# Block-masked Jacobi, identities added in VectorE's evictions, a one-product inverse, and another order of loads at the head

## The chip, the cores and the metric

One NeuronCore of a Trainium2 chip. Its engines are TensorE (PE; PEld is its weight load), VectorE (DVE), ScalarE (ACT), GpSimd (POOL) and SyncE (SP), each with its own queue of instructions in order, synchronised by semaphores. Time is device microseconds of one execution; lower is better.

## The reference

Three layers, one after the other, on 3072 tokens of width 384. The first is attention with a delta rule, 4 batches of 8 heads, 768 tokens, head dimension 48:

```python
k_n = k / (norm(k) + 1e-6)
for t in range(S):
    y[t] = q[t] @ state
    state = state + beta[t] * outer(k_n[t], v[t] - k_n[t] @ state)
```

Then a mixture of 8 experts (`argmax` of `x @ w_gate` picks one per token; `relu(x @ w1[e]) @ w2[e]`, scaled by a gate), and then `max(x @ w1, x @ w2, x @ w3) @ w_out` on every token.

## The kernel before

**Stages.** `attention_and_router` computes the delta rule, the router's logits and each token's place in a sorted list; `experts` runs over that list in tiles of 128 rows with a run-time number of tiles for each expert; `last_layer` runs over blocks of 512 rows.

**Attention in chunks.** The sequence is cut into chunks of 64 tokens. A step `k` (12 of them, `STEPS`) holds one pair of chunks for each of two streams (`st` 0 and 1, two batches), all 8 heads and two chunks at once: U = 8 blocks of 64x64 on each half of the partitions. For a chunk the recurrence is a triangular system, so each step and stream needs the inverse of I + a strictly triangular N of 64x64, for every head and chunk. It is made by the list `INV`:

- `kt`: transposes of the normalised keys; `gram`: products of keys with keys and queries (32 matmuls of 48x64 by 48x128), evicted by VectorE (L531) through `beta_mask` into `n_kb_a`; `split`: ScalarE casts N to 16 bits, `n_hi` (L483); `low`: GpSimd makes the rest, `n_lo` (L694).
- `jacobi` 0, 1, 2: T := mask(I + N T) within 4x4 blocks. TensorE (`diagonal`, L337) first puts the identity into PSUM with one pair of 64x512 matmuls, then sixteen 64x64 matmuls (`each_head`, L330) add N T; VectorE evicts through a mask (L535).
- `turn`: T transposed (ScalarE evicts, L486), and T put into the accumulator. `prod` and `update` 2 to 5: four doublings of the block size; VectorE evicts `p16` through a level's mask (L538), ScalarE evicts T and its transpose (L489, L491).
- `resid`: 2 pairs of `diagonal` (I and -T) and 32 small matmuls give I - T + N T, evicted by ScalarE (L494) to `p16`; `inv`: sixteen matmuls that copy T, transposed, into PSUM, a wait, and sixteen that add the correction; evicted by ScalarE to `t_inv` (L497).

`CHAIN` is what depends on the state of the chunk before: `ks`, `z`, `up` for each of two chunks, then `yt` (transpose), `lg` (logits, L454; VectorE copies them and picks the expert, L560 to L569), `rank` (L462, L463, the place among tokens of that expert), `slot`, and `send`, in which GpSimd scatters the rows of a tile to DRAM (L709).

**Order.** `walk` writes the order out by hand, the same for all engines: 16 slots per step; stream 1 runs `H` = 9 slots behind stream 0; `CHAIN` runs 17 slots behind `INV`. In slot 2 of step `k` stands stream 0's `split`, in slot 11 stream 1's. `NORM` prepares the keys of the next step: GpSimd squares them (`ksq`, L718), VectorE sums (L585), ScalarE takes roots (L517), VectorE inverts, GpSimd scales (`kn`, L685). Parts 10 to 12 convert a sixth of expert 0's weights each in steps 2 to 7 (L627, L638). Part 13, once, has GpSimd load expert 1's weights (L722).

**Queues at the head.** SyncE issues, in this order: keys of step 0 (`load_raw`, L274), `k_own` of step 0 (L279), `cf`, `beta`, `ch` (L289 to L291), queries and values of step 0, all loads of step 1, `wr` (L299), the first weights (L303), and the keys of step 2. TensorE, VectorE and GpSimd each wait for `const_in` 64, which the four constants make up together. In steps 2 to 11 SyncE also writes 14 blocks of zeros to `ys`, 192 KB each.

Of the kernel before, what the change touches and what calls it, by code (L numbers as in the profile page):

```python
# [16 lines left out]
P = 128  # L17
BATCH, HEADS, SEQ, D = 4, 8, 768, 48
DP = 64
C = 64  # L20
# [20 lines left out]
CF_IOTA = CF_BASE + C  # L41
# [8 lines left out]
CH_TRI = CH_REP + U * C  # L50
# [5 lines left out]
BLANK = MAXB - TILES  # L56
# [3 lines left out]
def constants():  # L60
# [10 lines left out]
    cf[:, CF_BASE:CF_BASE + C] = (row >> 2 == col >> 2) & (row >= col)  # L71
# [6 lines left out]
    ch[:, CH_REP:CH_REP + U * C] = np.tile(row == col, (1, U))  # L78
# [26 lines left out]
def attention_and_router(nc, ctx, sems, kt_in, kh, qh, vh, bh, cf_in, ch_in, wr_in, cf, ch, wr, routing, xs, ys, weights, w1, w2):  # L105
# [25 lines left out]
    n_lo = single("n_lo", [P, U, C], F16)  # L131
    t16 = single("t16", [P, U, C], F16)
# [10 lines left out]
    y_t = single("y_t", [P, KX, P], F32)  # L143
    best = sb("best", [P, 2], F32)
# [15 lines left out]
    const_in = sem("const_in")  # L160
    k_in = pair_of("k_in")
# [14 lines left out]
    n_lo_ready = pair_of("n_lo_ready")  # L176
    kb_ready = pair_of("kb_ready")
# [5 lines left out]
    updt_done = pair_of("updt_done")  # L183
    updtt_done = pair_of("updtt_done")
# [33 lines left out]
    ident_rep = ch[:, CH_REP:CH_REP + U * C]  # L218
# [8 lines left out]
    def mask_of(lv):  # L227

        at = CF_BASE if lv is None else CF_LV + (lv - LV0) * C
        return cf[:, at:at + C].unsqueeze(1).broadcast_to((P, U, C))  # L230
# [12 lines left out]
    NORM = {1: [0], 2: [1], 3: [2], 4: [10], 5: [3], 6: [4], 7: [5], 8: [6], 9: [7, 8], 10: [9], 12: [11], 13: [13], 14: [12]}  # L243
# [25 lines left out]
    def _(sp):  # L269
# [17 lines left out]
        for st in range(2):  # L287
            load_own(0, 0, st)
# [3 lines left out]
        for st in range(2):  # L292
            load_qv(0, 0, st)
        load_raw(1, 1)
# [22 lines left out]
        sp.wait_ge(zeroed, 16 * BLANK)  # L317
# [4 lines left out]
        sp.wait_ge(zeroed, 16 * BLANK + 16)  # L322

    @block.tensor
    def _(pe):
# [17 lines left out]
        def eye(s, u):  # L343
            return ident_rep[s, 0:C]

        def inv(k, par, st, what, lv):
            tb, ttb, pb = bank[st]
            n, nl, t, tt, pr = (lambda s, u, x=x[st]: x[s, u, :] for x in (n_hi, n_lo, t16, tt16, p16))
# [19 lines left out]
            elif what == "jacobi":  # L368
                if lv == 0:
                    pe.wait_ge(gram_out[st], 2 * k + 2)  # L370
                    pe.wait_ge(n_hi_ready[st], k + 1)
# [3 lines left out]
                diagonal(ident16, ident_rep, pb, True)  # L375
                each_head(n, eye if lv == 0 else t, pb).then_inc(jacobi_done[st], 1)
# [5 lines left out]
            elif what == "prod":  # L382
                if lv > LV0:
                    pe.wait_ge(t_out[st], LVS * k + lv - LV0)
                    pe.sem_inc(passed_pe, 1)
                each_head(n, t, pb, first=True).then_inc(prod_done[st], 1)
            elif what == "update":
# [3 lines left out]
                each_head(tt, pr, tb).then_inc(updt_done[st], 1)  # L391
                each_head(pr, tt, ttb).then_inc(updtt_done[st], 1)
            elif what == "resid":
# [3 lines left out]
                diagonal(ident16, ident_rep, pb, True)  # L397
                diagonal(neg16, flat(t16[st]), pb, False)
                each_head(n, t, pb)
                each_head(nl, t, pb).then_inc(resid_done[st], 1)  # L400
            elif what == "inv":
                pe.wait_ge(tt_out[st], (LVS + 1) * (k + 1))
                pe.sem_inc(passed_pe, 1)
                each_head(t, eye, ttb, first=True)
                pe.wait_ge(resid_out[st], k + 1)
                pe.sem_inc(passed_pe, 1)
                each_head(pr, tt, ttb).then_inc(inv_done[st], 1)

        def chain(k, par, st, what, e):
# [40 lines left out]
            elif what == "lg":  # L450
                pe.wait_ge(yt_out[st], k + 1)
                pe.sem_inc(passed_pe, 1)
# [13 lines left out]
        pe.wait_ge(const_in, 64)  # L466
# [7 lines left out]
    def _(act):  # L474
        def inv(k, par, st, what, lv):
# [11 lines left out]
            elif what == "update":  # L487
                act.wait_ge(updt_done[st], LVS * k + lv - LV0 + 1)
                act.copy(t16[st][:], tb).then_inc(t_out[st], 1)  # L489
                act.wait_ge(updtt_done[st], LVS * k + lv - LV0 + 1)  # L490
# [27 lines left out]

        act.wait_ge(blank, 1)
# [3 lines left out]
    def _(dve):  # L523
        def inv(k, par, st, what, lv):
# [8 lines left out]
            elif what == "jacobi":  # L533
                dve.wait_ge(jacobi_done[st], 3 * k + lv + 1)
                dve.tensor_tensor(t16[st][:], pb, mask_of(None), ALU.mult).then_inc(jacobi_out[st], 1)  # L535
            elif what == "prod":
                dve.wait_ge(prod_done[st], LVS * k + lv - LV0 + 1)
                dve.tensor_tensor(p16[st][:], pb, mask_of(lv), ALU.mult).then_inc(prod_out[st], 1)  # L538
# [41 lines left out]
        def norm(k, par, part):  # L580
# [26 lines left out]
            elif part == 9:  # L607
                dve.wait_ge(inv_norm, k + 1)
                if k >= 2:
# [42 lines left out]
        dve.wait_ge(const_in, 64)  # L652
        dve.tensor_copy(counted[:], ch[:, CH_AREA:CH_AREA + E])
# [24 lines left out]
    def _(pool):  # L678
        def inv(k, par, st, what, lv):
# [7 lines left out]
            elif what == "mask":  # L687
                if k >= 1:
                    pool.wait_ge(gram_out[st], 2 * k)
                pool.tensor_tensor(beta_mask[st][:], gp_mask.unsqueeze(1).broadcast_to((P, U, 2, C)),  # L690
                                   b.unsqueeze(2).unsqueeze(3).broadcast_to((P, U, 2, C)), ALU.mult).then_inc(beta_ready[st], 1)
            elif what == "low":
# [10 lines left out]
        def chain(k, par, st, what, e):  # L703
            if what == "send":
                to = 2 * k + st
                pool.wait_ge(slot_ready[st], k + 1)
                if k >= 1:
                    pool.wait_ge(rows_sent[st], 16 * k)
                pool.indirect_dma_start(xs, bass.IndirectOffsetOnAxis(ap=rows_at[:, to:to + 1], axis=0),  # L709
                                        y_tile[par][st][:], None).then_inc(rows_sent[st], 16)  # L710

        def norm(k, par, part):
# [6 lines left out]
            elif part == 13 and k == STEPS - 2:  # L719
                for i, w in enumerate((w1, w2)):  # L720
                    pool.wait_ge(weights.lo_ready[i], 1)
# [605 lines left out]
```

## Time and profile before

| | us |
|---|---|
| median of 3 runs | 1129.34 |
| lowest, highest | 1124.27, 1130.99 |
| the profiled execution | 1126.3 |
| its span, first to last instruction | 1124.6 |

| engine | busy us | share |
|---|---|---|
| TensorE matmul | 1025.3 | 91% |
| VectorE | 522.9 | 46% |
| ScalarE | 366.1 | 33% |
| GpSimd | 311.2 | 28% |

Attention runs from the head to about 510 us, the experts to about 860, the last layer to the end. Busy time on TensorE includes the drain of a matmul, which the next one overlaps; the distance between two starts is the better measure. A wait in brackets behind a row is idle time of that engine before it, with what ended it.

### The profile page before, as it was taken

The numbers are of one execution on the slowest core, as the hardware profiler recorded it, in microseconds if no ns is written. First come the engines' busy times: TensorE is split into PE (matmuls) and PEld (weight loads), VectorE is DVE, ScalarE is ACT, GpSimd is POOL, SyncE is SP. The second block draws the span as 40 slices with busy tenths as digits, with TensorE's granted clock in tenths as the row PEclk, the third lists the DMA queues.
The fourth block names the chain that finished last, engine by engine and source line by source line (L and its number), as shares of the span: only waits on it lengthen the run. The fifth ranks groups of instructions, "written<-read, shape, count | busy, mean of one in ns | idle before, by whom it ended". The sixth has DMA issues, their size and how long they took to land. (4 is left out here: it accounts for less than half of the span.)

```text
span 1124.6 us, 30958 instructions
## 1 busy us (share of the span) xinstructions
PE 1025.3 (91%) x13260; PEld 894.7 (80%) x13260; DVE 522.9 (46%) x1134; ACT 366.1 (33%) x730; POOL 311.2 (28%) x202
## 2 busy tenths in 40 slices
PE   0789989989999899975999999999599999999998
PEld 0677878878888788864999999998488888888888
DVE  4456666766666565525443444434242423232221
ACT  0245455545555455531222222222121212212111
POOL 2423433333334232103254555226310100000000
PEclk9999999999999999976999999999699999999999
DMA  8012122212221512002444344233201010100000
GB/s 273 16 31 77 41 73 66 70 56 84 62 79 40 196 34 64 17 15 93 154 167 169 130 160 152 105 124 115 72 27 36 22 43 14 42 21 22 15 15 29
DMA packets 58263, 84.90 MB, mean 75 GB/s; under 512 B 29088, under 2 KB 53024, under 8 KB 55584
## 3 DMA queue, kind: packets, MB, share of 16 engines
q1 hardware_dynamic: 52480, 46.94, 13.4%
q0 software_dynamic: 5664, 36.18, 9.4%
q8 instruction: 98, 1.61, 0.6%
q14 instruction: 21, 0.17, 0.1%
HBM read 61.67 MB, written 21.43 MB: 74 GB/s over the span
## 5 line engine op out<-in xcount | busy, mean ns | idle before, releaser
L1077 PE MATMUL hb<-early,last_h 128*128 128x512 f32 x648 | 208.2, 403 | 1.2 <-DVE early L1209 1.2
L1077 PEld LDWEIGHTS hb<-early,last_h 128*128 128x128 f32 x648 | 121.8, 191 | 29.4 <-DVE early L1209 1.6
L1077 PE MATMUL hb<-early,last_l 128*128 128x512 f32 x324 | 129.3, 399 | 0.0
L1215 DVE TENSOR_TENSOR m<-hb,m 128x512 f32<-128x512 f32 x36 | 24.9, 692 | 132.5 <-PE hb L1077 132.5
L330 PEld LDWEIGHTS bank<-t,n_hi 64*64 64x64 f16 x2688 | 65.9, 111 | 24.0 <-issue 8.5
L538 DVE TENSOR_TENSOR p<-bank,cf 128x512 f16<-128x512 f32 x96 | 66.0, 688 | 30.5 <-PE bank L330 29.6
L330 PE MATMUL bank<-t,n_hi 64*64 64x64 f16 x2688 | 72.7, 196 | 4.6 <-issue 3.7
L1077 PE MATMUL ob<-wo_h,early 128*128 128x384 f32 x288 | 75.2, 339 | 0.0
L1077 PEld LDWEIGHTS hb<-early,last_l 128*128 128x128 f32 x324 | 61.7, 190 | 15.1
L999 POOL TENSOR_TENSOR late<-w_raw,late 128x3072 fp32r<-128x3072 f32 x8 | 54.5, 6811 | 57.8 <-DVE late L939 57.5
L535 DVE TENSOR_TENSOR t<-bank,cf 128x512 f16<-128x512 f32 x72 | 49.7, 691 | 40.7 <-PE bank L330 40.0
L908 ACT CAST ht_h<-ht_bank 128x512 fp32r<-128x512 f32 x56 | 32.9, 587 | 109.3 <-PE ht_bank L862 55.4
L1110 POOL DMA_INDIRECT rows<-y_sorted,idx x24 | 23.0, 959 | 159.3 <-DVE scaled L1205 156.1
L489 ACT CAST t<-bank 128x512 f16<-128x512 f32 x96 | 56.3, 586 | 28.3 <-PE bank L330 26.2
L926 DVE TENSOR_TENSOR ht_l<-ht_bank,ht_h 128x512 fp32r<-128x512 f32 x56 | 38.7, 691 | 56.7 <-ACT ht_h L908 56.2
L790 PE MATMUL y_acc<-early,ht_h 128*128 128x384 f32 x240 | 63.8, 347 | 0.0
L709 POOL DMA_INDIRECT x_sorted<-y_tile,rows_at x24 | 24.4, 1017 | 128.7 <-DVE rows_at L577 127.3
L790 PE MATMUL h_bank<-early,xt_h 128*128 128x512 f32 x180 | 58.5, 407 | 1.4 <-DVE xt_l L921 1.3
L440 PE MATMUL chain<-z,n_kb_a 128*128 128x96 f32 x384 | 55.3, 287 | 3.4 <-issue 3.4
L491 ACT CAST tt<-bank 128x512 f16<-128x512 f32 x96 | 56.9, 593 | 0.9 <-PE bank L330 0.9
L685 POOL TENSOR_TENSOR kn<-k_raw,nrm 128x384 f32<-128x384 f32 x24 | 20.0, 834 | 133.2 <-DVE nrm L606 132.9
L421 PE MATMUL chain<-state,kq_t 128*128 128x96 f32 x384 | 55.2, 288 | 1.8 <-issue 1.6
(162 smaller groups left out, 2203.8 us busy)
## 6 DMA issues: line engine op xcount, KB each, us to landing
w_raw<-w POOLq DMA_DIRECT2D x14, 1536.0 KB, 7.6
kq_t<-qh SPq DMA_DIRECT2D x24, 256.0 KB, 3.4
y_sorted<-y_sb SPq DMA_DIRECT2D x31, 192.0 KB, 1.9
x_in<-x_sorted SPq DMA_DIRECT2D x29, 192.0 KB, 2.7
k_raw<-kt_in SPq DMA_DIRECT2D x24, 192.0 KB, 3.4
k_own<-kh SPq DMA_DIRECT2D x24, 192.0 KB, 3.2
v_in<-vh SPq DMA_DIRECT2D x24, 192.0 KB, 3.8
out<-o_sb SPq DMA_DIRECT2D x24, 192.0 KB, 1.8
```

What stands on the lines that cost most here:

```text
L330: ins = pe.matmul(out[s, C * u:C * u + C], lhs(s, u), rhs(s, u), start=first and u == 0, stop=True, skip_group_check=True)
L421: ins = pe.matmul(out[:, W * p:W * p + W], kq_t[par][st][:, NP * e + p, :, :].rearrange("q a t -> q (a t)"), state[st][:, p].rearrange("q ...
L440: ins = pe.matmul(out[:, W * p:W * p + W], n_kb_a[par][st][:, NP * e + p, 1:3, :].rearrange("q a t -> q (a t)"), z[st][:, p].rearrange("q ...
L489: act.copy(t16[st][:], tb).then_inc(t_out[st], 1)
L491: act.copy(tt16[st][:], ttb).then_inc(tt_out[st], 1)
L535: dve.tensor_tensor(t16[st][:], pb, mask_of(None), ALU.mult).then_inc(jacobi_out[st], 1)
L538: dve.tensor_tensor(p16[st][:], pb, mask_of(lv), ALU.mult).then_inc(prod_out[st], 1)
L790: ins = pe.matmul(out, a[x], b[y], start=first and i == 0, stop=last and i == 2)
L908: act.copy(ht[0][:, 4 * n:4 * n + 4].rearrange("p c t -> p (c t)"), ht_bank[n][:, :]).then_inc(ht_hi[n], 1)
L926: dve.tensor_tensor(ht[1][:, 4 * n:4 * n + 4].rearrange("p c t -> p (c t)"), ht_bank[n][:, :], ht[0][:, 4 * n:4 * n + 4].rearrange("p c t ...
L999: pool.tensor_tensor(splits[par][i][1], weights.flat_raw(i), splits[par][i][0], ALU.subtract).then_inc(weights.lo_ready[i], 1)
L1077: ins = pe.matmul(out, a[x], b[y], start=first and i == 0, stop=last and i == 2, skip_group_check=True)
```

## The change

- **Head.** `load_own` of step 0 goes behind the queries and values. `wr` gets a semaphore of its own, which only the first `lg` waits for, and `const_in` is waited for up to 48. GpSimd waits at its start for neither constants nor `blank`; its first `mask` waits for the constants. VectorE's wait for the constants and its copy into `counted` move to part 9 of step 0. ScalarE takes the root of a zero before anything else, so that its table is loaded.
- **Zeros.** The 14 writes to `ys` become one, issued ahead of the first weights. `BLANK` goes.
- **Expert 1's weights** are loaded by GpSimd behind the send of tile 22 (last step, stream 0) and no longer in part 13 of step 10.
- **Jacobi.** In `split`, GpSimd multiplies N by the mask of 4x4 blocks into a new 16-bit tile, `n_base`; the three rounds use it, without the identity products; VectorE's eviction adds the identity (from `cf`) and does not mask. `n_hi` is first waited for by `prod` 2. `CF_BASE` is the whole block mask.
- **Residual and inverse.** `resid` leaves out the identity product; VectorE, not ScalarE, evicts it and adds 2 I. `inv` is one set of sixteen products, of (2 I - T + N T) and T, without those that copied T.

```diff
@@ constants
+CF_EYE, CF_TWO: I and 2 I, 64 columns each; CH_REP shrinks from U*C to C columns
-    cf[:, CF_BASE:CF_BASE + C] = (row >> 2 == col >> 2) & (row >= col)
+    cf[:, CF_BASE:CF_BASE + C] = row >> 2 == col >> 2
...
@@ SyncE
         load_raw(0, 0)
-        for st in range(2):
-            load_own(0, 0, st)
         sp.dma_start(cf[:], cf_in).then_inc(const_in, 16)
         sp.dma_start(beta[:], bh).then_inc(const_in, 16)
         sp.dma_start(ch[:], ch_in).then_inc(const_in, 16)
         for st in range(2):
             load_qv(0, 0, st)
+        for st in range(2):
+            load_own(0, 0, st)
...
-        sp.dma_start(wr[:], wr_in).then_inc(const_in, 16)
+        sp.dma_start(wr[:], wr_in).then_inc(wr_in_sbuf, 16)
         sp.wait_ge(zeros_ready, 1)
+        sp.dma_start(ys[P * (LEAD + TILES):P * (LEAD + MAXB), :].rearrange("(n p) x -> p n x", p=P),
+                     zeros[:].unsqueeze(1).broadcast_to((P, MAXB - TILES, X))).then_inc(zeroed, 16)
...
-            for i in range(BLANK * (k - 2) // (STEPS - 2), BLANK * (k - 1) // (STEPS - 2)):
-                at = P * (LEAD + TILES + i)
-                sp.dma_start(ys[at:at + P, :], zeros[:]).then_inc(zeroed, 16)
@@ TensorE
             elif what == "jacobi":
                 if lv == 0:
                     pe.wait_ge(gram_out[st], 2 * k + 2)
-                    pe.wait_ge(n_hi_ready[st], k + 1)
+                    pe.wait_ge(n_base_ready[st], k + 1)
...
-                diagonal(ident16, ident_rep, pb, True)
-                each_head(n, eye if lv == 0 else t, pb).then_inc(jacobi_done[st], 1)
+                each_head(nb, eye if lv == 0 else t, pb, first=True).then_inc(jacobi_done[st], 1)
...
             elif what == "resid":
...
-                diagonal(ident16, ident_rep, pb, True)
-                diagonal(neg16, flat(t16[st]), pb, False)
+                diagonal(neg16, flat(t16[st]), pb, True)
                 each_head(n, t, pb)
                 each_head(nl, t, pb).then_inc(resid_done[st], 1)
             elif what == "inv":
                 pe.wait_ge(tt_out[st], (LVS + 1) * (k + 1))
-                pe.sem_inc(passed_pe, 1)
-                each_head(t, eye, ttb, first=True)
                 pe.wait_ge(resid_out[st], k + 1)
                 pe.sem_inc(passed_pe, 1)
-                each_head(pr, tt, ttb).then_inc(inv_done[st], 1)
+                each_head(pr, tt, ttb, first=True).then_inc(inv_done[st], 1)
...
-        pe.wait_ge(const_in, 64)
+        pe.wait_ge(const_in, 48)
@@ ScalarE
-            elif what == "resid":
-                act.wait_ge(resid_done[st], k + 1)
-                act.copy(p16[st][:], pb).then_inc(resid_out[st], 1)
...
+        act.wait_ge(zeros_ready, 1)
+        act.activation(root_of_zero[:], zeros[:, 0:1], ACT.Sqrt)
@@ VectorE
-                dve.tensor_tensor(t16[st][:], pb, mask_of(None), ALU.mult).then_inc(jacobi_out[st], 1)
+                dve.tensor_tensor(t16[st][:], pb, of_heads(CF_EYE), ALU.add).then_inc(jacobi_out[st], 1)
+            elif what == "resid":
+                dve.wait_ge(resid_done[st], k + 1)
+                dve.tensor_tensor(p16[st][:], pb, of_heads(CF_TWO), ALU.add).then_inc(resid_out[st], 1)
...
             elif part == 9:
                 dve.wait_ge(inv_norm, k + 1)
+                if k == 0:
+                    dve.wait_ge(const_in, 48)
+                    dve.tensor_copy(counted[:], ch[:, CH_AREA:CH_AREA + E])
@@ GpSimd
+            elif what == "split":
+                pool.wait_ge(gram_out[st], 2 * k + 2)
+                pool.tensor_tensor(n_base[st][:], n_kb_a[par][st][:, :, 0, :], of_heads(CF_BASE), ALU.mult).then_inc(n_base_ready[st], 1)
...
                                         y_tile[par][st][:], None).then_inc(rows_sent[st], 16)
+                if to == TILES - 2:
+                    for i, w in enumerate((w1, w2)):
+                        pool.wait_ge(weights.lo_ready[i], 1)
+                        pool.dma_start(weights.raw[i][:], w[1]).then_inc(weights.raw_again[i], 16)
...
-            elif part == 13 and k == STEPS - 2:
...
-        pool.wait_ge(const_in, 64)
-        pool.wait_ge(blank, 1)
```

## Rows read from the trace of the kernel before

**Rows 1.** A window of attention: length, busy of PE, PEld, DVE, ACT, POOL, PEclk, DMA.

```profile
235.00:265.00 30.00, 28.98 (x725) 25.10 (x720) 21.68 (x51) 16.08 (x35) 9.45 (x8) 1.00 0.28 80
```

**Rows 2.** Timeline of all engines, 0 to 50 us: start, us, engine, line, operation.

```profile
0.89 0.88 SPq L274 DMA_DIRECT2D k_raw<-kt_in  x2
...
14.99 0.43 SPq L299 DMA_DIRECT2D wr<-wr_in  x1
...
18.57 1.47 POOL L718 TENSOR_TENSOR ksq<-k_raw 128x768 f32<-128x768 f32 x1 [17.99 <-DMA wr<-wr_in]
...
21.11 1.28 ACT L517 ACT_TABLE_LOAD   x1 [21.11 <-DVE nrm L585]
...
25.19 1.08 PE L353 MATMUL bank<-cf,kn 128*128 128x128 f32 x4 [25.19 <-POOL kn L685]
...
27.05 3.67 PE L365 MATMUL bank<-kq_t 48*64 48x128 f32 x32 [0.77 <-ACT kq_t L479]
```

**Rows 3.** DMA of 0 to 25 us: traffic, then issues with KB and us to landing.

```profile
DMA packets 6739, 7.44 MB, mean 298 GB/s; under 512 B 4566, under 2 KB 6230, under 8 KB 6486
...
k_raw<-kt_in SPq DMA_DIRECT2D x5, 192.0 KB, 2.5
...
ch<-ch_in SPq DMA_DIRECT2D x1, 258.0 KB, 5.9
```

**Rows 4.** Timeline of VectorE: the key sums of three steps.

```profile
289.32 0.94 DVE L585 TENSOR_REDUCE nrm<-ksq 128x16 f32<-128x768 f32 x1
...
361.27 0.94 DVE L585 TENSOR_REDUCE nrm<-ksq 128x16 f32<-128x768 f32 x1
...
403.19 0.94 DVE L585 TENSOR_REDUCE nrm<-ksq 128x16 f32<-128x768 f32 x1
```

**Rows 5.** Timeline of TensorE in one step, 200 to 235 us.

```profile
205.66 0.38 PE L337 MATMUL bank<-ch 64*64 64x512 f16 x2
205.88 0.41 PE L330 MATMUL bank<-t,n_hi 64*64 64x64 f16 x16
206.22 0.84 PE L454 MATMUL chain<-wr,y_t 128*128 128x16 f32 x6
206.99 0.44 PE L330 MATMUL bank<-ch,t 64*64 64x64 f16 x16
207.27 0.42 PE L330 MATMUL bank<-tt,p 64*64 64x64 f16 x16
...
208.78 0.17 PE L462 MATMUL chain<-chosen,ch 128*128 128x8 f16 x1 [0.37 <-DVE chosen L569]
```

**Rows 6.** Timeline of all engines around stream 1's first Jacobi round.

```profile
195.99 1.96 PE L365 MATMUL bank<-kq_t 48*64 48x128 f32 x32
...
197.19 1.50 DVE L531 TENSOR_TENSOR n_kb_a<-bank,beta_mask 128x512 f32<-128x512 f32 x2 [0.40 <-PE bank L365]
...
200.63 0.63 ACT L483 CAST n_hi<-n_kb_a 128x512 f16<-128x512 f32 x1
...
201.35 1.15 POOL L694 TENSOR_TENSOR n_lo<-n_kb_a,n_hi 128x512 f16<-128x512 f32 x1 [4.49 <-ACT n_hi L483]
201.36 0.40 PE L337 MATMUL bank<-ch 64*64 64x512 f16 x2 [0.43 <-issue]
```

**Rows 7.** Windows around the load of expert 1's weights (columns as in Rows 1).

```profile
385.00:390.00 5.00, 1.73 (x45) 1.51 (x38) 0.69 (x1) 1.17 (x3) 1.90 (x2) 1.00 0.99 402
390.00:395.00 5.00, 4.83 (x102) 4.17 (x101) 2.18 (x8) 1.06 (x2) 0.00 (x0) 0.62 0.44 122
```

**Rows 8.** Timeline of all engines, 379 to 393 us.

```profile
390.18 0.35 PE L440 MATMUL chain<-z,n_kb_a 128*128 128x96 f32 x2 [3.44 <-issue]
```

**Rows 9.** Timeline of GpSimd: the send of tile 22.

```profile
498.23 0.97 POOL L709 DMA_INDIRECT x_sorted<-y_tile,rows_at  x1 [9.58 <-DVE rows_at L577]
```

**Rows 10.** Instructions on `w_raw`, 60 to 540 us: ns min/median/max, first and last start.

```profile
L939 DVE CAST late<-w_raw x2: 1760/2382/3003, 521.2 to 528.6; 128x3072 fp32r<-128x3072 f32 x2
...
DMA to landing us min/median/max: 7.0/7.8/11.2
```

More of the change, by code:

```diff
@@ L40 @@
 CF_BASE = CF_LV + (LEVELS - 2) * C
-CF_IOTA = CF_BASE + C
+CF_EYE = CF_BASE + C
+CF_TWO = CF_EYE + C
+CF_IOTA = CF_TWO + C
 CF_STEP = CF_IOTA + E
@@ L49 @@
 CH_REP = CH_NEG + P
-CH_TRI = CH_REP + U * C
+CH_TRI = CH_REP + C
 CH_ONE = CH_TRI + P
@@ L55 @@
 LEAD = 3
-BLANK = MAXB - TILES
 AREA = TILES + MINB
@@ L70, in constants @@
         cf[:, CF_LV + (lv - 2) * C:CF_LV + (lv - 1) * C] = below & ((col >> lv) == (row >> lv) - 1)
-    cf[:, CF_BASE:CF_BASE + C] = (row >> 2 == col >> 2) & (row >= col)
+    cf[:, CF_BASE:CF_BASE + C] = row >> 2 == col >> 2
+    cf[:, CF_EYE:CF_EYE + C] = row == col
+    cf[:, CF_TWO:CF_TWO + C] = 2.0 * (row == col)
     cf[:, CF_IOTA:CF_IOTA + E] = E - np.arange(E)
@@ L77, in constants @@
     ch[:, CH_NEG:CH_NEG + P] = -np.eye(P)
-    ch[:, CH_REP:CH_REP + U * C] = np.tile(row == col, (1, U))
+    ch[:, CH_REP:CH_REP + C] = row == col
     ch[:, CH_TRI:CH_TRI + P] = np.arange(P)[:, None] < np.arange(P)[None]
@@ L131, in attention_and_router @@
     n_lo = single("n_lo", [P, U, C], F16)
+    n_base = single("n_base", [P, U, C], F16)
     t16 = single("t16", [P, U, C], F16)
@@ L160, in attention_and_router @@
     const_in = sem("const_in")
+    wr_in_sbuf = sem("wr_in_sbuf")
     k_in = pair_of("k_in")
@@ L176, in attention_and_router @@
     n_lo_ready = pair_of("n_lo_ready")
+    n_base_ready = pair_of("n_base_ready")
     kb_ready = pair_of("kb_ready")
@@ L225, in attention_and_router, with of_heads @@
     rows = [slice(C * hh, C * hh + D) for hh in range(2)]
-    def mask_of(lv):
-        at = CF_BASE if lv is None else CF_LV + (lv - LV0) * C
+    def of_heads(at):
         return cf[:, at:at + C].unsqueeze(1).broadcast_to((P, U, C))
@@ L343, in eye @@
         def eye(s, u):
-            return ident_rep[s, 0:C]
+            return eye16[s, :]
         def inv(k, par, st, what, lv):
             tb, ttb, pb = bank[st]
-            n, nl, t, tt, pr = (lambda s, u, x=x[st]: x[s, u, :] for x in (n_hi, n_lo, t16, tt16, p16))
+            n, nl, nb, t, tt, pr = (lambda s, u, x=x[st]: x[s, u, :] for x in (n_hi, n_lo, n_base, t16, tt16, p16))
             if what == "kt":
@@ L384, in inv @@
                     pe.wait_ge(t_out[st], LVS * k + lv - LV0)
-                    pe.sem_inc(passed_pe, 1)
+                else:
+                    pe.wait_ge(n_hi_ready[st], k + 1)
+                pe.sem_inc(passed_pe, 1)
                 each_head(n, t, pb, first=True).then_inc(prod_done[st], 1)
@@ L451, in chain @@
                 pe.wait_ge(yt_out[st], k + 1)
+                if k == 0 and st == 0:
+                    pe.wait_ge(wr_in_sbuf, 16)
                 pe.sem_inc(passed_pe, 1)
@@ L718, in norm @@
                 pool.tensor_tensor(ksq[:], keys, keys, ALU.mult).then_inc(squares, 1)
-            elif part == 13 and k == STEPS - 2:
-                for i, w in enumerate((w1, w2)):
-                    pool.wait_ge(weights.lo_ready[i], 1)
-                    pool.dma_start(weights.raw[i][:], w[1]).then_inc(weights.raw_again[i], 16)
-        pool.wait_ge(const_in, 64)
-        pool.wait_ge(blank, 1)
         run(lambda a, c, b, n: walk(a, c, b, n, inv, chain, norm))
```

29 lines of the change are left out of this document (14 added, 15 removed).

## The prediction

> **What bounds the kernel now.** I read the page's engine shares first, then the windows of 30 us through the attention stage, then the timeline of all engines at the head, the timeline of TensorE inside one steady step, and the waits that are left. The page gives TensorE 91% of the span (table above), and a window in the middle of attention has it busy for 28.98 of 30 us, VectorE 21.68, ScalarE 16.08 [rows 1]. So TensorE sets the pace there, and what an edit is worth is the distance between starts on TensorE, not the printed duration: a group of sixteen 64x64 matmuls prints 0.41 to 0.44 us but the next one starts 0.28 to 0.34 us later [rows 5]. At the head it is otherwise: nothing is multiplied until 25.19 us, because GpSimd's first square waits 17.99 us for the last of the constant loads, `wr`, issued at 14.99 behind the data of steps 0 and 1 [rows 2]. From there the work is one dependent chain. The third thing is a single hole: at 390.18 TensorE had waited 3.44 us inside a group of matmuls for nothing that the profile names ("issue"), while the DMA engines were 0.99 busy, and afterwards the clock stood at a mean of 0.62 for 5 us [rows 7, 8], a mix of its levels 1.2 and 2.4 GHz.
>
> **The head.** Two loads of keys are issued by 1.77 us [rows 2] and land a median 2.5 us later [rows 3], so about 4.3; the added freedom is that GpSimd waits for nothing else. Before, the first square began at 18.57 and the first transpose at 25.19, 6.62 us of chain. The table load of the root, 1.28 us of it, now runs while the keys arrive (zeros are written early, ScalarE is idle). That leaves 5.34 us: TensorE could start at 4.3 + 5.3 = 9.6. It also waits for three constants now: their issues (0.43 us each, as the row of `wr` has it) follow the keys at once, so the last, `ch`, is issued near 3.2 and lands 5.9 us later [rows 3], at about 9.1, in time. I take 9.9 us, a gain of 15.3; bounds 12 (constants late behind traffic, 13 us) to 16.
>
> **What that start runs into.** Up to 25 us the queue moved 7.44 MB at a mean of 298 GB/s [rows 3]. One write of 14 x 192 KB = 2.75 MB of zeros is added ahead of the first weights (and taken from later steps): 9.2 us more at that rate, so the DMA engines are full until about 34 us, and the first inversion now runs under that, from 10 us. Its data (queries, values, the keys of step 1) are issued ahead of the zeros, the keys of step 2 are wanted a whole step later. What can suffer is TensorE's own instruction supply. The nearest row is the hole of 3.44 us under a full DMA [rows 8]; the chain is sparse here, since it waits for evictions, so I charge 2 us, bounds 0 and 7 (two such holes).
> The Trainium skill (Runtime: NRT & Kernel Launch, Instruction fetch mechanics) says that instructions come in blocks by the sequencer's own DMA queue and that crossing a block is mostly hidden. By that rule this term would be 0; the row of 3.44 us speaks for a cost when the engines are full.
>
> **The weights of expert 1.** Their two loads leave the tenth step and go behind the send of tile 22, at 498.23 before [rows 9]; they land 7.0 to 11.2 us after issue, so by about 510, and VectorE first reads them at 521.2 [rows 10]. What follows them on GpSimd's queue is only the last send. Cost 0 to 2 us if that send lands late, I take 0.5. What goes is the hole: the marks of VectorE's key sums stand at 289.32, 361.27 and 403.19 [rows 4]: two steps of 35.98 and then one of 41.92, so the step with the loads cost 5.9 more. I take all of it; bounds 3 and 6. The remaining zero writes also leave the steps, one or two of 192 KB each; I take 2 us for shorter refill holes, bounds 0 and 6.
>
> **The inversion on TensorE.** Per step and stream: each of three Jacobi rounds loses a pair of 64x512 products with the identity, the residual loses one such pair, and the inverse loses the sixteen products that copied T. A pair takes 205.88 - 205.66 = 0.22 us of TensorE's order, the sixteen 207.27 - 206.99 = 0.28 us [rows 5]. That is 4 x 0.22 + 0.28 = 1.16 us, and with 12 steps and 2 streams 27.8 us. Not all of it is the end's to have:
> - The sixteen stand between the logit products and the rank product, which at 208.78 waits for VectorE's choice of expert (0.37 us [rows 5]). VectorE's work from the logits on is not shorter, so what is taken ahead of the wait only lengthens it. I count these 0.28 at nothing: 24 x 0.28 = 6.7 us lost, 21.1 left.
> - The residual's eviction moves from ScalarE to VectorE; two evictions take 1.50 there [rows 6], so 0.75 us more, twice a step, on an engine busy 21.68 of 30 [rows 1]. What is queued behind it is the third Jacobi eviction and then the logits' copy, whose choice the rank product waits for. In the steps with weight pieces I charge 0.5, in the others 0.1: 3.5 us in all; bounds 0 and 0.75 x 24 = 18.
> - The Jacobi rounds take a masked N that GpSimd makes (1.15 us, by the row of n_lo, an operation of the same size) where ScalarE's copy took 0.63 [rows 6]. But ScalarE got to it late: in stream 1 the masked Gram was ready at 197.19 + 1.50 = 198.69, the copy ran at 200.63, and TensorE stood 0.43 us [rows 6]. GpSimd can start at once (its next task is queued behind): 198.8 + 1.15 = 199.95, ahead of TensorE's arrival near 200.9. That takes away about 0.6 us of distance in eleven steps, 6.6 us. In stream 0 the two paths come out equal. A GpSimd that is late by a mask or a send would lose 1 to 2 us a step instead; bounds: gain 7, loss 12; I take a gain of 4.
> - Additions in the evictions cost what the multiplications by a mask did: same engine, same operands.
>
> So attention gains 21.1 - 3.5 + 4 = 21.6 us in the stage; in the first chain, where latency counts, the pairs leave too and GpSimd's 0.5 us longer mask comes in, which is within these numbers. Behind attention nothing is changed but the counts of a semaphore.
>
> **The sum** is 15.3 - 2 + 5.9 - 0.5 + 2 + 21.6 = 42.3 us. The profiled execution took 1126.3 us (its span is 1124.6); less the sum, 1084.0. The median of the runs is 1129.34, 3 us above; the same sum from there is 1087.0. I put the forecast between, at 1086. About 1% (11 us) is what a measurement of this kernel can tell from no change.
>
> **Rivals.**
> - *TensorE's time goes, but the waits take it.* With VectorE busy 21.68 of 30 us and every eviction in order behind another, the stage could keep its steps: only 8 us of the 21.6 come through. Then 1126.3 - 15.3 + 2 - 5.9 - 8 - 1.5 = 1098. For it: only a few waits in a steady step are at zero margin, and they are VectorE's; against it: groups follow each other at their shortest distance nearly everywhere.
> - *The full DMA at the head starves the first chain.* Two or three holes of 3.44 us and late constants: the head yields 5 instead of 13.3, giving 1094; for it the row of the hole, against it that before, too, loads were behind loads and landed in 2.5 to 5.9 us.
> - *The holes and the clock's dips were worse than counted.* If the refill holes leave with the zeros and no dip follows, and TensorE's 27.8 us come through whole: about 1071.
> - *Slower: the clock.* The head already shows the lower level: 32 Gram products took 3.67 us at 27.05 [rows 2] against 1.96 at 195.99 [rows 6], half rate, while TensorE waited for evictions; and after the hole it fell again [rows 7]. The change removes the widest products and leaves the waits. If TensorE fell to 1.2 GHz in attention, a step of 36 us with 29/30 of it on TensorE would grow by up to 35 us; 1.2 such steps, one in ten, eat the whole sum, and three give 1126.3 - 42.3 + 105 = 1189. Against it: a window of 28.98 busy us of 30 held the level 1.00 [rows 1], and 2 us less of a 36 us step leave it at nine tenths.
> The Trainium skill (TensorE: Matmul & The Clock Gate, HAM oscillation) warns of just this: idle stretches between products send the engine to half rate. The trace agrees after the hole; whether shorter waits suffice, no row of the steady steps shows.
>
> **Chances.** The forecast's case (1076 to 1093) 0.56, waits take it (1093 to 1106) 0.16, a starved head 0.12, better than counted (1066 to 1076) 0.11, the clock or something that turns it around 0.05, of which 0.02 land within 1%. Range 1069 to 1104: it takes in a starved head and most of the waits, and leaves out the tails of both sides. Faster by over 1% (under 1118) 0.95, within 1% 0.02, slower 0.03.
>
> **What would show it.** The first transpose near 10 us and no later than 13; the key-sum marks of VectorE 34 to 35 us apart with no step near 42; no 64x512 identity pair in the Jacobi rounds; the first Jacobi group without a wait on stream 1; the rank product waiting longer (0.6 us or more) than 0.37; the first read of expert 1's weights without a wait. A mark spacing still over 36 us would say that the waits took the gain; Gram groups of 3.7 us outside the first 40 us would say the clock.

## The result, and the profile after

The changed kernel takes 1169.64 us (median of 4, 1159.48 to 1184.01) against 1130.16 us: a ratio of 1.032, interval 1.021 to 1.044. It is slower; the forecast was 1086, and the whole range 1069 to 1104 lay on the wrong side. One of the four, 1184.01 us, was a slow execution, and the mean of the other three is 1166.3, so differences from this kernel are known to about 13 us only. The profiled execution has a span of 1157.3 us.

The page of the changed kernel: span, busy time of two engines in 40 slices, the granted clock in tenths, and the group of GpSimd's new operation.

```profile
span 1157.3 us, 29818 instructions
...
PE   4798878988989989984999999999599999999999
...
DVE  5666776776766767643544344344242314242321
...
PEclk9977888887799989986899999999789999999999
...
L703 POOL TENSOR_TENSOR n_base<-n_kb_a,cf 128x512 f16<-128x512 f32 x24 | 30.8, 1284 | 199.4 <-DVE n_kb_a L534 199.4
```

The clock is what leaps out: under nine tenths in most slices of attention (the first 19), where TensorE has 576 matmuls fewer. The head did what it should. Timeline of all engines, the lines that answer to [rows 2]:

```profile
3.90 1.47 POOL L734 TENSOR_TENSOR ksq<-k_raw 128x768 f32<-128x768 f32 x1 [3.31 <-DMA k_raw<-kt_in]
...
9.31 1.09 PE L357 MATMUL bank<-cf,kn 128*128 128x128 f32 x4 [9.31 <-POOL kn L692]
```

15.9 us earlier than before. All of that is given back, and more, between 50 and 440 us: the third key sum comes at 49.18 us (62.79 before), the twelfth at 435.55 (403.19 before), so that 46 us are lost between them. Some of VectorE's key sums, which answer to [rows 4]:

```profile
227.06 0.94 DVE L591 TENSOR_REDUCE nrm<-ksq 128x16 f32<-128x768 f32 x1
...
271.64 0.94 DVE L591 TENSOR_REDUCE nrm<-ksq 128x16 f32<-128x768 f32 x1
...
319.05 0.94 DVE L591 TENSOR_REDUCE nrm<-ksq 128x16 f32<-128x768 f32 x1
...
359.34 0.94 DVE L591 TENSOR_REDUCE nrm<-ksq 128x16 f32<-128x768 f32 x1
...
394.99 0.94 DVE L591 TENSOR_REDUCE nrm<-ksq 128x16 f32<-128x768 f32 x1
```

Steps of 44.6, 47.4, 40.3 and 35.7 us, where the same four took 38.1, 36.2, 36.5 and 35.4 before. Windows of 50 us (busy of PE, PEld, DVE, ACT, POOL, then the clock; columns as in [rows 1]):

```profile
100.00:150.00 50.00, 43.34 (x877) 38.31 (x877) 34.30 (x74) 19.35 (x41) 15.51 (x13) 0.77 0.17 48
...
250.00:300.00 50.00, 43.80 (x861) 38.89 (x856) 34.82 (x74) 18.99 (x41) 16.62 (x14) 0.76 0.16 44
...
350.00:400.00 50.00, 46.21 (x1097) 41.19 (x1098) 35.94 (x88) 24.97 (x55) 19.91 (x18) 0.97 0.18 53
```

A mean of 0.76 is half the time at 1.2 GHz and half at 2.4. The one step of 35.7 us lies where the clock held (1.00 from 359 to 395 us). So two questions: what made TensorE wait, and what the clock adds.

The timeline of all engines (weight loads left out), right behind stream 1's Gram products, answers to [rows 6]:

```profile
203.87 1.94 PE L369 MATMUL bank<-kq_t 48*64 48x128 f32 x32
...
205.07 1.49 DVE L534 TENSOR_TENSOR n_kb_a<-bank,beta_mask 128x512 f32<-128x512 f32 x2
...
206.47 3.34 DVE L626 TENSOR_TENSOR beta_k<-nrm,beta 64x8 f32<-64x8 f32 x4
206.63 1.30 POOL L703 TENSOR_TENSOR n_base<-n_kb_a,cf 128x512 f16<-128x512 f32 x1 [3.77 <-DVE n_kb_a L534]
...
207.89 1.90 POOL L699 TENSOR_TENSOR beta_mask<-cf,beta 128x1024 f32<-128x1024 f32 x1
...
208.62 0.42 PE L334 MATMUL bank<-ch,n_base 64*64 64x64 f16 x16
...
209.84 0.71 DVE L561 TENSOR_TENSOR state<-state,chain 64x192 f32<-64x192 f32 x2
...
210.65 0.52 PE L450 MATMUL chain<-cf,y_tile 128*128 128x128 f32 x3 [1.61 <-issue]
...
211.42 0.44 PE L334 MATMUL bank<-p,tt 64*64 64x64 f16 x16 [0.25 <-DVE p L544]
```

GpSimd makes the masked N at once, as forecast, and the first Jacobi group starts without a wait. But VectorE's next work is `beta_k`, four products of 64x8 elements from two SBUF tiles, 0.17 us each when alone. Here the four take 3.34 us: they end when GpSimd's mask of N and then `beta_mask`, which stands behind it, have ended (207.89 + 1.90 = 209.79). In the kernel before the same four took 0.68 us, because GpSimd had made that `beta_mask` well ahead of the Gram's eviction:

```profile
193.80 1.90 POOL L690 TENSOR_TENSOR beta_mask<-cf,beta 128x1024 f32<-128x1024 f32 x1
...
198.60 0.68 DVE L617 TENSOR_TENSOR beta_k<-nrm,beta 64x8 f32<-64x8 f32 x4
```

The new operation waits for VectorE's eviction of the Gram (3.77 us in the row at 206.63), and all that GpSimd has behind it in its queue now runs beside what VectorE does next. In the changed kernel the state's update waits behind `beta_k`, `yt` waits for the state, and TensorE stands 1.61 us (put down to "issue", but VectorE's row at 209.84 is what it needed) and 0.25 more. The groups of VectorE that were held, over attention, changed kernel:

```profile
L626 DVE TENSOR_TENSOR beta_k<-nrm,beta 64x8 f32<-64x8 f32 x48 | 39.3, 818 | 0.5
...
L636 DVE CAST early<-w_raw 128x512 fp32r<-128x512 f32 x12 | 19.7, 1682 | 0.0
L647 DVE TENSOR_TENSOR early<-w_raw,early 128x512 fp32r<-128x512 f32 x12 | 17.1, 1423 | 0.0
```

and the kernel before:

```profile
L638 DVE TENSOR_TENSOR early<-w_raw,early 128x512 fp32r<-128x512 f32 x12 | 15.0, 1247 | 0.0
...
L617 DVE TENSOR_TENSOR beta_k<-nrm,beta 64x8 f32<-64x8 f32 x48 | 11.1, 232 | 0.5
...
L627 DVE CAST early<-w_raw 128x512 fp32r<-128x512 f32 x12 | 4.5, 418 | 0.0
```

VectorE loses 28.2 + 15.2 + 2.1 = 45.5 us by being held. The Trainium skill (SBUF — State Buffer, Who interferes with whom) states the rule: an instruction of VectorE with two SBUF inputs contends with one of GpSimd that reads SBUF, and a copy or cast in a two-port mode contends with GpSimd too; whichever is issued first has the shared ports for the whole instruction, and the other is blocked. The trace agrees: 0.68 us for four against 3.34, and 0.42 us for a cast against 1.68.

### The profile page after: what moved, and what is told of

Read it like the earlier page. It is cut to its first block and busy times, and to the rows that moved or that the text cites. A ratio compares the mean times of both kernels' runs of the same rounds, so it can differ in the third digit from the quotient of the medians.

```text
span 1157.3 us, 29818 instructions
## 1 busy us (share of the span) xinstructions
PE 1043.1 (90%) x12684; PEld 917.5 (79%) x12684; DVE 579.5 (50%) x1158; ACT 353.6 (31%) x707; POOL 340.3 (29%) x226
## 5 line engine op out<-in xcount | busy, mean ns | idle before, releaser
L703 POOL TENSOR_TENSOR n_base<-n_kb_a,cf 128x512 f16<-128x512 f32 x24 | 30.8, 1284 | 199.4 <-DVE n_kb_a L534 199.4
L423 PE MATMUL chain<-state,kq_t 128*128 128x96 f32 x384 | 67.3, 330 | 0.9 <-issue 0.4
L553 DVE TENSOR_TENSOR rhs<-v_in,chain 64x192 f32<-64x192 f32 x96 | 33.4, 348 | 68.4 <-PE chain L423 66.9
L334 PEld LDWEIGHTS bank<-t,n_hi 64*64 64x64 f16 x1920 | 51.2, 119 | 19.0 <-issue 12.8
L918 ACT CAST ht_h<-ht_bank 128x512 fp32r<-128x512 f32 x56 | 32.9, 587 | 109.3 <-PE ht_bank L872 55.4
L334 PE MATMUL bank<-tt,p 64*64 64x64 f16 x1920 | 57.9, 203 | 7.4 <-issue 7.2
L334 PE MATMUL bank<-t,n_hi 64*64 64x64 f16 x1920 | 58.4, 205 | 5.3 <-issue 3.6
L423 PEld LDWEIGHTS chain<-state,kq_t 128*128 128x128 f32 x384 | 59.6, 237 | 2.8 <-issue 1.2
L442 PE MATMUL chain<-z,n_kb_a 128*128 128x96 f32 x384 | 60.5, 306 | 0.0
L538 DVE TENSOR_TENSOR t<-bank,cf 128x512 f16<-128x512 f32 x72 | 49.4, 686 | 22.0 <-PE bank L334 21.4
```

Of the source, the lines that this page charges most:

```text
L334: ins = pe.matmul(out[s, C * u:C * u + C], lhs(s, u), rhs(s, u), start=first and u == 0, stop=True, skip_group_check=True)
L423: ins = pe.matmul(out[:, W * p:W * p + W], kq_t[par][st][:, NP * e + p, :, :].rearrange("q a t -> q (a t)"), state[st][:, p].rearrange("q ...
L442: ins = pe.matmul(out[:, W * p:W * p + W], n_kb_a[par][st][:, NP * e + p, 1:3, :].rearrange("q a t -> q (a t)"), z[st][:, p].rearrange("q ...
L538: dve.tensor_tensor(t16[st][:], pb, of_heads(CF_EYE), ALU.add).then_inc(jacobi_out[st], 1)
L553: dve.tensor_tensor(rhs[st][s, :, hh, :], v_in[par][st][s, e], by_head[0:C, hh], ALU.subtract).then_inc(rhs_out[st], 1)
L918: act.copy(ht[0][:, 4 * n:4 * n + 4].rearrange("p c t -> p (c t)"), ht_bank[n][:, :]).then_inc(ht_hi[n], 1)
```

## The experiments

Theory P: GpSimd's added operation holds VectorE up, and TensorE waits. Theory C: without the identity products TensorE does too little and its clock falls. All medians below were taken beside runs of the kernel before, at 1127.6 to 1129.2 us.

**Head and moves alone**

```diff
  the head, the zeros and the load of expert 1's weights as in the change; the inversion as before
```

> The kernel before with the new head, the one write of zeros and the later load of expert 1's weights; the inversion as before. Both theories (P: GpSimd's new mask of N holds VectorE up through two-input operations; C: TensorE loses its clock because the identity products are gone) say that nothing of the loss is here: first transpose near 9.3 us (15.9 less), the step with the 3.44 us hole 6 less, clock as before: 1130 - 20 = 1106 to 1112 us. A third theory, H (the early, sparse start and the full DMA bring the clock down), says above 1130.

1107.66 us, ratio 0.979 (0.973 to 0.985). So nothing of the loss is here, H is out, and the terms of the sum for these parts, 20.7 us, hold together: 21.5. Not each of them does; see the section on the prediction. This kernel is the base of the next ones.

**Jacobi alone**

```diff
  base, and
-                diagonal(ident16, ident_rep, pb, True)
-                each_head(n, eye if lv == 0 else t, pb).then_inc(jacobi_done[st], 1)
+                each_head(nb, eye if lv == 0 else t, pb, first=True).then_inc(jacobi_done[st], 1)
  GpSimd's n_base, VectorE's eviction + I
```

> The head and moves as in the run beside it, and of the inversion only the Jacobi part: GpSimd's masked N, no identity products in the three rounds, identity added in VectorE's eviction; residual and inverse as before. P: VectorE's beta_k operations take 0.7 us each as in the changed kernel and the time is near that of it, 1150 to 1170. C: three of the four pairs are gone, so most of the clock loss too, 1150 to 1170, but with beta_k back at 0.25 us. If it is the residual's eviction on VectorE (theory V): 1090 to 1100.

1173.79 us, 66 above the base and no faster than the whole change. `beta_k` took 0.80 us each, so this is P, with or without C. The loss is all in the Jacobi part.

**Residual and inverse alone**

```diff
  base, and the residual evicted by VectorE with 2 I, one pair and the sixteen copy products out
```

> The kernel of 1107.66 us, with only the residual and the inverse changed: one pair and the sixteen copy products less, the residual evicted by VectorE. P: GpSimd has nothing new, so 1098 to 1107. C: one pair less of four: 1100 to 1115. If the eviction on VectorE is what costs (V): 1115 to 1125.

1104.02 us, 3.6 below the base, with both at some us of spread: no loss, and little of the 24 x (0.22 + 0.28) = 12 us that TensorE was spared. V is out. (The prediction's terms for this part are 24 x 0.22 - 3.5 = 1.8 us.)

**GpSimd's operation alone**

```diff
  base, and
+            elif what == "split":
+                pool.wait_ge(gram_out[st], 2 * k + 2)
+                pool.tensor_tensor(n_base[st][:], n_kb_a[par][st][:, :, 0, :], base mask, ALU.mult)
```

> The kernel of 1107.66 us, with only GpSimd's masked copy of N added, which nothing reads and nobody waits for; TensorE's work as before. P: VectorE's beta_k goes from 0.19 to 0.8 us, TensorE waits 1 to 4 us more in each step and the time is 1135 to 1165. C, or that it is the Jacobi rounds' wait for GpSimd: no change, 1105 to 1112.

1147.33 us: 39.7 us for an operation that nobody waits for, 24 times. Groups of VectorE:

```profile
L626 DVE TENSOR_TENSOR beta_k<-nrm,beta 64x8 f32<-64x8 f32 x48 | 38.5, 802 | 0.5
L636 DVE CAST early<-w_raw 128x512 fp32r<-128x512 f32 x12 | 19.6, 1676 | 0.0
```

P is shown without any edit on TensorE. But the clock fell here too, with all the identity pairs in place. A window of 50 us:

```profile
100.00:150.00 50.00, 45.10 (x954) 39.11 (x956) 34.37 (x74) 21.01 (x44) 15.50 (x13) 0.81 0.18 49
```

In the four windows from 50 to 250 us it was 0.93, 0.81, 0.85 and 0.83, which is 58 us at 1.2 GHz. So up to 29 of the 39.7 us can be the clock's, brought down by the waits. Under "Jacobi alone" the mask is made by GpSimd as well, but three of the four pairs are out and the rounds wait for the mask: there 16 us less of work on TensorE went with 26 us more of time.

**The same, with `beta_k` moved**

```diff
-    NORM = {... 9: [7, 8], 10: [9], 12: [11], 13: [13], 14: [12]}
+    NORM = {... 9: [7, 8], 12: [11], 14: [12], 15: [9]}
```

> The 1147.33 us kernel (old inversion, GpSimd makes a masked N that nobody reads), with beta_k moved from slot 10 to 15. If the collision with beta_k is what it costs: beta_k at 0.2 us and 1108 to 1120 (1107.66 without the extra operation; the weight casts are still held in steps 2 to 7). If the extra operation costs by its presence: above 1130.

1126.44 us (median of ten; one of them took 2457.6 us, the others 1122.11 to 1130.78), 21 of the 40 us back, less than expected. The clock of the profiled run went from 0.946 to 0.971. The rest lies in the steps with weight pieces:

```profile
L647 DVE TENSOR_TENSOR early<-w_raw,early 128x512 fp32r<-128x512 f32 x12 | 22.9, 1905 | 0.0
L636 DVE CAST early<-w_raw 128x512 fp32r<-128x512 f32 x12 | 19.6, 1675 | 0.0
L626 DVE TENSOR_TENSOR beta_k<-nrm,beta 64x8 f32<-64x8 f32 x48 | 9.2, 192 | 0.5
```

The casts stay held and the remainders even more (1.91 us for 1.19 in the base). By VectorE's key sums five of these six steps take 41 to 42 us and the later ones 35.4 to 36.3. So the collisions, with `beta_k` and with the weight pieces, are the cost. That the operation's presence alone is not, the run called "Both" below shows best: there GpSimd makes the mask, all collisions are moved and the pairs stand, and the time is 1108.52 us, 0.9 above the base (it is spared the sixteen copy products, which with a pair were worth 3.6 us in the run above).

**The change, with `beta_k` moved**

```diff
  the changed kernel with part 9 of NORM in slot 15
```

> The changed kernel (1169.64 us), with only beta_k moved from slot 10 to slot 15; the weight casts stay at 4, 12 and 14. P, and mostly by beta_k (39.3 us of the 45 that VectorE lost): beta_k back at 0.2 us, 1130 to 1145, most of the 40 us that all the shifts gave. If the casts count as much: 1145 to 1160, and in the steps without weight pieces no change against the run with all shifts.

1126.57 us: one small group, moved by five slots, gives 43 us (40 from the mean of 1166.3). It is more than expected. The clock of the profiled run is 0.950, against 0.926.

**The change, with all colliding operations moved**

```diff
-    NORM = {... 4: [10], ... 8: [6], 9: [7, 8], 10: [9], 12: [11], 14: [12]}
+    NORM = {... 8: [6, 10], 9: [7, 8], 14: [11], 15: [12, 9]}
```

> The changed kernel, with VectorE's operations that read two SBUF tiles or copy from SBUF moved to slots in which GpSimd has run out of work: beta_k from slot 10 to 15, the weight casts from 4 to 8, the weight remainders from 12 and 14 to 14 and 15. Nothing is added to TensorE. P: beta_k falls from 0.8 to 0.2 us, the clock comes back to 0.97 and the time to 1085 to 1105. C: VectorE is freed but the clock still falls in ten places: 1140 to 1165.

1129.75 us, neither theory's number, and no better than with `beta_k` alone, though the casts are back at 0.42 us and the remainders at 0.68. Why the casts' freedom bought nothing in the median is open. The ten executions lie between 1119.76 and 1132.68 us, and the profiled one, 1119.99 with a clock of 0.962, is among the quickest. In it the waits of 2 to 3.3 us behind the casts (last section) are gone, but two holes stand inside groups of matmuls, for nothing that the profile names, and each step with one took 42.4 us where its neighbours took 37.2 to 39.5:

```profile
248.48 0.58 PE L334 MATMUL bank<-tt,p 64*64 64x64 f16 x14 [3.32 <-issue]
...
327.56 0.37 PE L334 MATMUL bank<-p,tt 64*64 64x64 f16 x6 [3.17 <-issue]
```

**The change, with the pairs back**

```diff
+                diagonal(ident16, ident_rep, pb, True)
                 each_head(nb, eye if lv == 0 else t, pb, first=True).then_inc(jacobi_done[st], 1)
```

> The changed kernel, with the four pairs of 64x512 identity products per step and stream put back at their old places, ahead of the groups that overwrite them: TensorE's work as before save for the sixteen copy products. C: the granted clock comes back to 0.97 and the time falls to 1100 to 1115. P: VectorE is still held (beta_k 0.8 us), TensorE waits as much and has 21 us more to do in the full-clock stretches: 1165 to 1185, at best 1150 if part of the clock comes back.

1155.10 us: with VectorE held as much as before (0.80 us), 21 us of extra work on TensorE did not make the kernel slower. By the medians it is 14.5 us faster, by the means (1166.3 and 1156.7) 9.6, which is not clear of the spread; P alone said 1165 to 1185. The clock went from 0.926 to 0.955.

**Both**

```diff
  all colliding operations moved, and the four pairs back at their old places
```

> The changed kernel with both: VectorE's operations in the slots of the run with shifted operations, and the four pairs of identity products back. So far VectorE freed gave 40 us and the pairs, with VectorE still held, 14 us though they cost 21. P alone true: the pairs cost 15 to 20 here, 1140 to 1150. P and C both: the clock holds at 0.97 and the time is 1095 to 1110.

1108.52 us, 21 below the same without the pairs. The clock of the profiled run is 0.975, and its longest hole in the steps is 1.6 us.

**The pairs inside the waits**

```diff
+                    diagonal(ident16, ident_rep, ttb, True)
                     pe.wait_ge(n_base_ready[st], k + 1)
...
+                    diagonal(ident16, ident_rep, ttb, True)
                     pe.wait_ge(jacobi_out[st], 3 * k + lv)
...
+                diagonal(ident16, ident_rep, ttb, True)
                 pe.wait_ge(resid_out[st], k + 1)
```

> The kernel with shifted operations, and four pairs of identity products per step and stream again, but written to a bank that nobody reads and issued ahead of the waits for the Jacobi evictions and for the residual's. C: TensorE does what it did in the 1108.52 us kernel, part of it in time that it would have waited, the clock holds at 0.97 and the time is 1095 to 1108. If the clock had only to do with the length of the waits between real products: 1115 to 1140.

1096.87 us, ratio 0.974 (0.969 to 0.980). 32.9 us faster than the same kernel without these products, which nobody reads. Two windows of 50 us:

```profile
100.00:150.00 50.00, 47.58 (x1154) 41.70 (x1155) 35.04 (x92) 24.71 (x54) 22.73 (x19) 1.00 0.20 58
...
250.00:300.00 50.00, 46.05 (x1124) 39.77 (x1124) 32.72 (x90) 24.98 (x54) 21.77 (x18) 1.00 0.20 58
```

and the two lowest of the kernel without them, all colliding operations moved:

```profile
250.00:300.00 50.00, 45.74 (x1029) 40.90 (x1028) 32.47 (x89) 22.12 (x47) 16.06 (x15) 0.92 0.15 45
300.00:350.00 50.00, 44.41 (x998) 39.51 (x996) 27.89 (x73) 23.12 (x49) 21.81 (x18) 0.86 0.20 58
```

Full clock in all eight windows from 50 to 450 us, against 0.86 to 1.00: without these products TensorE spent 33 us of the 400 at 1.2 GHz, most of it right behind the two holes shown above, one just ahead of the first of these windows and one in the second. The kernel with them has no such hole (the longest wait is 1.6 us). So the products and the full clock go together, but half of 33 us is the most that the rate can explain of the 32.9; the holes and the other waits make up the rest, and why the holes are gone isn't shown.

**Only the pairs out**

```diff
  base, and
-                diagonal(ident16, ident_rep, pb, True)
  in the three rounds and the residual, the next product with first=True
```

> The kernel of 1107.66 us (new head and moves, old inversion), with only the four pairs of identity products per step and stream left out, so the identity is missing from T and from the residual; VectorE, GpSimd and ScalarE do what they did. C: the clock falls in several places, below 0.965, and the 21 us of TensorE's order do not come through: 1100 to 1125. P: the clock stays at 0.97 and the time is 1086 to 1095.

1095.07 us, 12.6 below the base, of 21 that TensorE was spared; clock 0.970, against 0.972 for the base. The identity is missing, so this kernel's results are not the reference's; it has the same instructions save for the pairs, and in the profiles the gain lies in attention (twelfth key sum at 373.25 us, in the base at 386.33). This sits at the edge of P's range. Where VectorE isn't held and gets nothing new, the pairs can leave without a loss of clock. So C, as I had put it, is too strong: the missing products cost only together with waits.

**The mask on VectorE**

```diff
             elif what == "split":
-                pool.tensor_tensor(n_base ...)
+                dve.tensor_tensor(n_base ...)
```

> The changed kernel (1169.64 us), with the masked N made by VectorE in slot 2 in place of GpSimd; VectorE's other operations in their old slots. P: nothing new on GpSimd, so beta_k at 0.2 us, and VectorE has 24 x 0.7 = 17 us more: 1100 to 1125, with some dips of the clock left. C alone: dips as in the changed kernel, 1150 to 1175.

1109.17 us (0.986, 0.981 to 0.991). The same arithmetic as the change, 60 us faster, although VectorE has 24 x 0.69 = 17 us of work more: P again, from the other side. Since nothing holds it, VectorE is busy for 546 us in all, against 580.

**The mask on VectorE, the pairs inside the waits**

> The changed kernel with the masked N made by VectorE and the four pairs of identity products, which nobody reads, issued ahead of the waits. Without the pairs it took 1109.17 us, with 34 us at the lower clock in the steps. C: none or one such stretch in the steps, and 1088 to 1102. If the clock does not hang on TensorE's work: 1105 to 1125.

1095.59 us, ratio 0.972 (0.968 to 0.976). One window with the pairs and, in the second fence, without:

```profile
200.00:250.00 50.00, 48.41 (x1197) 42.82 (x1191) 38.10 (x105) 26.23 (x57) 17.46 (x15) 1.00 0.22 64
```

```profile
200.00:250.00 50.00, 42.52 (x995) 37.57 (x995) 31.94 (x86) 21.46 (x46) 13.14 (x11) 0.92 0.21 61
```

The second window holds the one long hole of that kernel, 3.60 us inside a group of matmuls, put down to "issue"; with the pairs there is none. Over the eight windows the kernel without the pairs was at 1.2 GHz for 31 us, the one with them not at all. With the run of 1096.87 us, from which it can't be told apart, this is the fastest kernel that computes everything, 3% under the kernel before.

**Old Jacobi, new residual, operations moved**

> The 1104.02 us kernel (new head and moves, new residual and inverse, Jacobi as before), with VectorE's operations in the shifted slots. P says that the collisions were small there already (beta_k 0.21, remainders 1.25 us): the remainders fall to 0.7, and 1 to 6 us come of it, 1098 to 1103.

1104.77 us against 1104.02: no difference, and just outside the 1098 to 1103 expected, although the remainders fell from 1.25 to 0.68 us. In that kernel their 0.6 us held up nothing that set the time.

## Why the prediction was wrong

- **Head: right.** 9.31 us for a forecast of 9.9; the gain 15.9 for 15.3. The full DMA behind it was charged at 2 us; the second and third key sums lie 32.6 us apart in the base kernel and 31.4 before, so 1.2.
- **Expert 1's weights and the zeros: right in their sum with the head, 21.5 us for 20.7 by the medians (by the interval 17 to 30), but not term by term.** No hole of 3.44 us is left. Yet the step that had it went from 41.9 to 39.5 us in the base kernel, 2.4 for a forecast of 5.9 and under its bound of 3: in that step a wait of 1.35 us at 357.69 is followed by some 7 us at 1.2 GHz. Of the 2 us for the zeros nothing shows: from the third to the eleventh key sum the steps take 298.7 us, 298.5 before. By the profiled executions all these parts gave 18.1 us, of which 16.9 by the twelfth key sum. The charge for TensorE's instruction supply was not tested on its own.
- **GpSimd's masked N: the step that failed.** The forecast was "GpSimd can start at once ... I take a gain of 4", with a bound of 12 us of loss by a late mask. It was at once, and TensorE's own wait did vanish. What I did not do is ask what VectorE does in that moment: I named what is queued behind the operation on GpSimd, but not that the operation's wait would shift it, nor who shares its way into SBUF. The measured effect of the operation alone is +39.7 us, in place of 4 less. How much of that is its own 1.3 us and how much is `beta_mask`, shifted by its wait, no run separates. The sign was in the trace of the kernel before: of the two remainders in a step one took 1.81 us and the other 0.68.
- **The clock: the rival was right in kind, not in cause, and priced at 5%.** "The change removes the widest products and leaves the waits" is half of it. The waits were not left, they were made (by VectorE), and in seven of the eight windows of 50 us between 50 and 450 us the mean clock was 0.76 to 0.90. The step with full clock took 35.7 us; five with 0.75 to 0.88 took 43.6 to 47.4. Those five also have weight pieces, whose held casts cost waits of their own: with `beta_k` moved in the old inversion, such steps took 41 to 42 us at 0.96 to 1.00. Over the eight windows the mean is 0.856, so TensorE was at 1.2 GHz for (1 - 0.856) x 2 x 400 = 115 us. Half of that, 58 us, is the most that the lower rate itself can have cost: 1.6 steps of 36 us, against the breakeven of 1.2 that I had set. The base has 17 us at 1.2 GHz in the same windows.
- **Parts do not add.** From the base: GpSimd's operation +39.7, pairs out -12.6, residual and inverse -3.6, in sum 1131; measured 1169.6. That counts the gain of the residual's pair twice, so the sum is nearer 1134, and with the mean of 1166.3 the excess is 32. The 32 to 38 us over are what holding VectorE and sparing TensorE cost together: +66 for the Jacobi part alone, and -43 by moving `beta_k`, more than GpSimd's operation costs in the base.
- **The inversion's gain, 21.6 us: mis-sized even where nothing is held.** Without the pairs and with nothing else changed, 12.6 of 21.1 us came through. That leans to the first rival ("the waits take it", 8 us); that the rest went into waits for VectorE is likely, not shown.

What stays open: how much of the 32 to 38 us is the clock and how much are waits that only exist when TensorE is early; why freeing the weight casts bought nothing once `beta_k` was out of the way; and where the holes of 3.2 to 3.6 us inside groups of matmuls come from. They stand in two kernels whose TensorE has the very instructions of the changed one, which has none longer than 1.7 inside a group; the DMA engines were 0.68 to 0.71 busy in the 5 us before or around their start.

## What to carry to other kernels

Before an operation goes to GpSimd, list what VectorE runs in the same stretch, and what stands behind the operation in GpSimd's queue, which its wait will shift. Here VectorE's operations with two SBUF inputs and its casts from SBUF stood until GpSimd was done (3.34 us for 0.68, 1.68 for 0.42), and all that was queued behind them stood too. Work taken from TensorE gave 12.6 of its 21 us where nothing else changed, and less than nothing where VectorE was held at the same time. So check the granted clock by windows before and after. Products that nobody reads, put ahead of a wait, can be cheaper than the wait: twice they took the time down, by 32.9 and 13.6 us.

## What the runs showed of the hardware

Waits of 1.4 to 3.3 us were enough to bring TensorE to 1.2 GHz again and again. The waits of TensorE of the changed kernel between 50 and 450 us (what was waited for: us in total, times, longest):

```profile
PE bank L334 <- DVE t L538: 19.6, 12, 3.3
PE chain L450 <- issue: 14.2, 9, 1.6
PE bank L334 <- issue: 9.6, 11, 1.7
PE bank L334 <- DVE p L544: 3.9, 15, 0.3
```

The long ones, 2 to 3.3 us, are those of `turn` for the third Jacobi eviction (L538), one in each of the six steps with weight pieces. That eviction stands behind the two held casts:

```profile
95.45 3.53 DVE L636 CAST early<-w_raw 128x512 fp32r<-128x512 f32 x2
...
99.63 0.69 DVE L538 TENSOR_TENSOR t<-bank,cf 128x512 f16<-128x512 f32 x1
...
100.47 0.63 PE L334 MATMUL bank<-ch,t 64*64 64x64 f16 x16 [3.26 <-DVE t L538]
```

Each of the four windows of 50 us from 100 to 300 us holds at least one, and the clock there was 0.76 to 0.86. The waits of 1.4 to 1.6 us (L450) are those of `yt`, behind the held `beta_k`. They bring the clock down too; here are the windows around the one that ends at 210.65:

```profile
205.00:210.00 5.00, 4.04 (x97) 3.49 (x93) 4.82 (x8) 2.57 (x6) 3.22 (x3) 1.00 0.01 3
210.00:215.00 5.00, 4.10 (x62) 3.44 (x64) 4.96 (x7) 1.85 (x4) 3.54 (x3) 0.72 0.50 136
215.00:220.00 5.00, 5.00 (x109) 4.55 (x106) 3.37 (x11) 1.25 (x3) 0.00 (x0) 0.50 0.00 0
```

Between 50 and 450 us the clock fell fifteen times: six times during a long wait or within 1.3 us of its end, six times 1 to 2 us after the end of one of 1.4 to 1.6 us, and three times with no wait over 0.8 us in the 5 us before. It doesn't fall after each: the three that end at 164.54, 344.77 and 382.36 were not followed by a fall within 5 us. In the same view of the kernel with its mask on GpSimd and the pairs ahead of the waits, the longest is 1.6 us:

```profile
PE bank L335 <- issue: 11.6, 16, 1.6
PE bank L335 <- DVE t L542: 3.6, 10, 0.8
```

There the clock was 1.00 in all eight windows. Nor does TensorE's busy time of a window tell which way it goes: with `beta_k` moved in the old inversion it was busy for 43.11 of the 50 us from 50 to 100 us, at a clock of 1.00, and in the changed kernel for 43.34 of 50, at 0.77. The Trainium skill (TensorE: Matmul & The Clock Gate, HAM oscillation) ties a fall of the clock to idle gaps between products, there waits for DMA. The trace agrees that gaps do it, at 2 to 3.3 us; here waits of 1.4 to 1.6 us for VectorE did it as well.
